# A gated linear-attention, MLP and gated-convolution kernel: a new step order, the first mask level as a product, and another place for the second phase's first split

## The reference

```python
f = 1 / (1 + exp(-f_logit))
for t in range(S):                                   # attention, per head
    state = f[:, :, t, :, None] * state + outer(k[:, :, t], v[:, :, t])
    y[:, :, t] = q[:, :, t] @ state
xn = (x - mean(x)) / sqrt(var(x) + 1e-6) * g_ln      # MLP on the 384 channels of y
x  = x + relu(xn @ w_ch1) @ w_ch2                    # 384 -> 1536 -> 384
h  = relu(x @ w_in)                                  # 384 -> 1024
gate = sigmoid(conv_w[0]*h[t-1] + conv_w[1]*h[t] + conv_w[2]*h[t+1])
out = (h * gate) @ w_out                             # 1024 -> 384
```

## Time and profile before

| | us |
|---|---|
| median of 3 runs | 750.89 |
| lowest, highest | 747.57, 751.74 |
| the profiled execution's own time | 746.53 |
| its span, first to last instruction | 744.8 |

### The profile page before, as it was taken

The page is one execution under the profiler, slowest core; times in us unless marked ns, Lnnn a source line. Parts: engine busy times, 40 slices in busy tenths (PEclk is TensorE's granted clock), DMA queues, the critical chain, the costliest instruction groups (busy, mean ns, idle before and its releaser), DMA issues.

```text
span 744.8 us, 20447 instructions
## 1 busy us (share of the span) xinstructions
PE 706.2 (95%) x8912; PEld 652.2 (88%) x8912; DVE 544.8 (73%) x1003; ACT 312.2 (42%) x604; POOL 182.2 (24%) x179
## 2 busy tenths in 40 slices
PE   3789999999999998999999999999999999999998
PEld 3556798998998998999899899999989999999997
DVE  4878989889769868858867974532577777767774
ACT  3244531431431251251143143222467776776764
POOL 8102303264154344327306414400000000000000
PEclk9758999999999999999999999999999999999999
DMA  6825601561433244073152112114310220220101
GB/s 191 196 72 151 140 3 55 157 144 55 81 148 95 41 143 140 2 181 87 56 150 85 56 55 86 54 36 151 106 54 1 74 73 1 74 70 4 37 37 37
DMA packets 22793, 62.90 MB, mean 84 GB/s; under 512 B 4240, under 2 KB 15248, under 8 KB 22704
## 3 DMA queue, kind: packets, MB, share of 16 engines
q1 hardware_dynamic: 22704, 61.60, 29.0%
HBM read 52.14 MB, written 9.45 MB: 83 GB/s over the span
## 4 chain that ended last, share of the span: by engine, by line
PE 65%; DMA 12%; DVE 10%; POOL 7%; issue 3%; SPq 2%; ACT 1%; DVEq 0%; POOLq 0%; ACTq 0%
DMA NEAR<-near 10%; PE bank L1287 9%; PE bank L1289 9%; PE bank L1288 9%; PE bank L1092 9%; PE bank L1094 8%; PE bank L1093 7%; PE bank L1004 6%; DVE AT L820 3%; DVE Q L797 2%; POOL NEAR L588 2%; POOL NEAR L603 2%; PE bank L1044 2%; POOL NEAR L590 1%; POOL NEAR L586 1%
## 5 line engine op out<-in xcount | busy, mean ns | idle before, releaser
L688 ACT ACTIVATE HHI<-bank 128x384 fp32r<-128x384 f32 x96 | 46.9, 490 | 171.3 <-PE bank L1094 171.1
L1264 DVE SCALAR_TENSOR_TENSOR TB<-HB,CW,TB 128x440 f32<-128x440 f32 x112 | 75.9, 677 | 47.0 <-ACT TB L1227 45.0
L1092 PE MATMUL bank<-HHI,W2H 128*128 128x384 f32 x288 | 103.8, 361 | 0.0
L1092 PE MATMUL bank<-XH,W1H 128*128 128x384 f32 x288 | 102.1, 355 | 0.7 <-ACT W2L L708 0.7
L1094 PE MATMUL bank<-HHI,W2L 128*128 128x384 f32 x288 | 97.4, 338 | 0.0
L1093 PE MATMUL bank<-HLO,W2H 128*128 128x384 f32 x288 | 97.0, 337 | 0.0
L1094 PE MATMUL bank<-XH,W1L 128*128 128x384 f32 x288 | 96.7, 336 | 0.0
L1093 PE MATMUL bank<-XL,W1H 128*128 128x384 f32 x288 | 96.5, 335 | 0.0
L1004 PEld LDWEIGHTS bank<-Q,K 48*64 48x64 f32 x3840 | 66.6, 145 | 30.9 <-issue 30.8
L915 DVE SCALAR_TENSOR_TENSOR HLO<-bank,HHI 128x384 fp32r<-128x384 f32 x96 | 53.2, 555 | 50.4 <-ACT HHI L688 49.3
L1004 PE MATMUL bank<-Q,K 48*64 48x32 f32 x3840 | 71.3, 229 | 18.3 <-DVE Q L797 12.6
(11 more groups left out here) (130 smaller groups left out, 1430.8 us busy)
## 6 DMA issues: line engine op xcount, KB each, us to landing
NEAR<-near SPq DMA_DIRECT2D x21, 960.0 KB, 5.0
V<-v SPq DMA_DIRECT2D x8, 576.0 KB, 9.0
x2d<-X SPq DMA_DIRECT2D x8, 576.0 KB, 4.5
F<-f SPq DMA_DIRECT2D x14, 288.0 KB, 5.1
K<-k SPq DMA_DIRECT2D x14, 288.0 KB, 5.7
Q<-q SPq DMA_DIRECT2D x14, 288.0 KB, 7.4
XB<-x2d SPq DMA_DIRECT2D x6, 663.0 KB, 5.8
out<-OB SPq DMA_DIRECT2D x6, 660.0 KB, 4.5
```

The costliest lines, as they stand in the source:

```text
L688: nc.scalar.activation(HHI[:, g % RA], ub[g % 2][:, 0:T], ACT.Relu).then_inc(hh_ready, 1)
L1092: mm(dst, ah, bh, start=start, stop=False, **kw)
L1264: nc.vector.scalar_tensor_tensor(out=TB[:, g % RB], in0=HB[:, g % RB, tap:tap + TB_], scalar=CW[:, g, tap:tap + 1], in1=TB[:, g % RB], op0 ...
```

## The change

Four things. The PERIOD list is reordered on all engines but SyncE, with the same 141 steps; START has a few steps in other places (on TensorE the first y now stands ahead of the first ktr). The first level's mask of every unit but unit 0, and the diagonal step of unit 0, are written as a product of the scores with the mask (`tensor_tensor`, multiply) and no longer as a predicated copy; the tiny memset ahead of each of these goes. In LAST the seven `wb` steps stand among the steps 14 to 42 and no longer 24 to 50, and `xb` stands eight steps earlier. TensorE's wait at the start of the second phase asks for the three pieces of W3 only; for all seven pieces it waits ahead of the first `down`.

```diff
         PERIOD = steps("""
-            hlo0 near0 up0 hhi0 up1 ktr0 hlo1 xacc0 xacc1 up2 xacc2 up3 nsum0 down0 gates0 hhi1 gates1
...
+            hhi0 up0 hlo0 near0 nsum0 up1 hlo1 xacc0 ktr0 up2 baseK0 xacc1 xacc2 hlo2 y0 down0 xadd0 up3
...
-        LAST = (up_down[:24] + merge(up_down[24:], [("wb", j) for j in range(len(nxt.WJ))])
-                + [("xb", 0), ("down", G1 - 1)] + [("xout", d) for d in range(KT)])
+        LAST = (up_down[:14] + merge(up_down[14:42], [("wb", j) for j in range(len(nxt.WJ))]) + [("xb", 0)] + up_down[42:]
+                + [("down", G1 - 1)] + [("xout", d) for d in range(KT)])
...
# self_(p): the diagonal of unit 0
-                spare = 2 * MASKED + NC + p.ahead
-                nc.vector.memset(SPARE[:, spare:spare + 1], 0.0)
...
-                        ins = nc.vector.copy_predicated(to, part.broadcast_to([HALF, p.n * NP, 2, QUARTER]), of)
+                        ins = tt(to, of, part.broadcast_to([HALF, p.n * NP, 2, QUARTER]), ALU.mult)
...
# mask(p, i)
-                    spare = st + (MASKED + NC) * p.ahead
-                    nc.vector.memset(SPARE[:, spare:spare + 1], 0.0)
+                    if st or u.first:
+                        spare = st + (MASKED + NC) * p.ahead
+                        nc.vector.memset(SPARE[:, spare:spare + 1], 0.0)
...
-                    ins = nc.vector.copy_predicated(to, part.broadcast_to([HALF, p.n * NP, QUARTER // m, m]), of)
+                    spread_mask = part.broadcast_to([HALF, p.n * NP, QUARTER // m, m])
+                    if st or u.first:
+                        ins = nc.vector.copy_predicated(to, spread_mask.bitcast(I32), of)
+                    else:
+                        ins = tt(to, of, spread_mask, ALU.mult)
...
# tensor(pe) of phase_b
-            pe.wait_ge(wbl_ready, len(carried.WJ))
+            pe.wait_ge(wbl_ready, KT)
...
                 if t.first and g == 0:
+                    pe.wait_ge(wbl_ready, len(carried.WJ))
                     pe.wait_ge(x2_ready, KT * (NU + 1))
```

More of the change, by code:

```diff
@@ L214, in phase_a @@
         VE = sb("VE", [P, NC])
-        SPARE = sb("SPARE", [P, 2 * MASKED + NC + 2])
+        SPARE = sb("SPARE", [P, 2 * MASKED + NC])
         RSTD = sb("RSTD", [P, NC])
@@ L322, in phase_a @@
         PERIOD = steps("""
-            hlo0 near0 up0 hhi0 up1 ktr0 hlo1 xacc0 xacc1 up2 xacc2 up3 nsum0 down0 gates0 hhi1 gates1
[L324 to L330, removed]
+            hhi0 up0 hlo0 near0 nsum0 up1 hlo1 xacc0 ktr0 up2 baseK0 xacc1 xacc2 hlo2 y0 down0 xadd0 up3
+            baseQ0 down1 hhi1 up4 ktok0 neary0 pT0 down2 hhi2 kv0 score0 pQ0 gates0 hlo3 up5 down3 sscale0
+            hlo4 st0 gates1 ktr1 up6 hhi3 mask0 hhi4 mask1 near1 hhi5 hlo5 nsum1 ktok1 pK1 pT1 norm0 hhi6 y1
+            neary1 hlo6 pQ1 xadd1 down4 sscale1 hhi7 norm1 xn0 up7 st1 pow0 pK2 xh0 sscale2 pT2 near2 kv1
+            score1 pow1 hlo7 neary2 xl0 up8 hhi8 mask2 xnt0 mask3 ktok2 down5 up9 down6 pQ2 nsum2 hlo8 mask4
+            ktr2 score2 hhi9 mask5 pK3 xadd2 pT3 xn1 y2 down7 pQ3 norm2 hlo9 st2 pK4 pT4 hhi10 pQ4 hlo10
+            up10 kv2 xl1 pK5 xn2 score3 pT5 up11 copy3 xh1 pQ5 hlo11 copy4 hhi11 down8 xh2 copy5 xnt1 xl2
+            pow2 pK6 score4 down9 xout0 pT6 xout1 down10 xnt2 pQ6 xout2 score5 down11
             """)
@@ L364, in phase_a @@
             score4.0 copy4.a wsub7.0 score5.a wlo6.0 score5.0 copy4.0 wsub8.0 mask3.0 copy5.a copy5.0 pQ2.0
-            baseK0.1 pQ3.a pK3.0 ktr0.0 mask5.a y0.0 mask4.0 pT3.0 ktok0.0 mask5.0 pQ3.0 pK4.a wlo7.0
+            baseK0.1 pQ3.a y0.0 mask4.0 pK3.0 ktr0.0 mask5.a pT3.0 ktok0.0 mask5.0 pQ3.0 pK4.a wlo7.0
             wsub9.0 ktr1.0 kv0.0 xadd0.0 ktok1.0 wlo8.0 wlo9.0 baseQ0.1 score0.1 pT4.a pK4.0 wsub10.0 pQ4.a
@@ L373, in phase_a @@
             down1.0 xl1.0 sscale2.0 score5.1 up4.0 pK3.1 xh2.0 down2.0 xl2.0 mask4.1 wlo15.0 pT3.1 ktr0.1
-            mask5.1 down3.0 st2.0 y0.1 pQ3.1 wlv8.0 hlo0.0 hlo1.0 hhi0.0 score0.2 pK4.1 hhi1.0 pT4.1 kv0.1
+            mask5.1 down3.0 st2.0 y0.1 pQ3.1 wlv8.0 hlo0.0 hhi0.0 hlo1.0 score0.2 pK4.1 hhi1.0 pT4.1 kv0.1
             wlv9.0 whi9.0 pQ4.1 hlo2.0 baseK0.2 down4.0 ktr1.1 wlv10.0 whi10.0 up5.0 pK5.1 pT5.1 azero0.2
             y1.1 copy3.1 whi11.0 pQ5.1 neary1.1 up6.0 baseQ0.2 hhi2.0 pK6.1 pT6.1 copy4.1 score1.2 copy5.1
-            down5.0 pQ6.1 hhi3.0 hlo3.0 wlv11.0 kv1.1 pT0.2 pQ0.2 hlo4.0 sscale0.1 hhi4.0 ktok0.1 xadd0.1
+            down5.0 pQ6.1 hhi3.0 hlo3.0 wlv11.0 hlo4.0 kv1.1 pT0.2 pQ0.2 sscale0.1 hhi4.0 ktok0.1 xadd0.1
             pK1.2 ktok1.1 hhi5.0 hhi6.0 up7.0 st0.1 hhi7.0 pT1.2 nsum1.1 pQ1.2 up8.0 down6.0 mask0.2
@@ L755, in self_ @@
                 dve.wait_ge(odd_done[p.ahead], 1)
-                spare = 2 * MASKED + NC + p.ahead
-                nc.vector.memset(SPARE[:, spare:spare + 1], 0.0)
                 for g in range(2):
                     rows = slice(HALF * g, HALF * g + HALF)
-                    part = SELF[rows, QUARTER * g:QUARTER * g + QUARTER].bitcast(I32)
+                    part = SELF[rows, QUARTER * g:QUARTER * g + QUARTER]
                     part = part.rearrange("p n two -> p two n").unsqueeze(1)
@@ L808, in mask @@
                     dve.wait_ge(score_done[p.ahead], u.count(LEVELS, st + 1))
-                    spare = st + (MASKED + NC) * p.ahead
-                    nc.vector.memset(SPARE[:, spare:spare + 1], 0.0)
+                    if st or u.first:
+                        spare = st + (MASKED + NC) * p.ahead
+                        nc.vector.memset(SPARE[:, spare:spare + 1], 0.0)
                 m = 2 << st
                 rows = slice(HALF * g, HALF * g + HALF)
-                part = MASK[rows, st, QUARTER * g:QUARTER * g + QUARTER].bitcast(I32)
+                part = MASK[rows, st, QUARTER * g:QUARTER * g + QUARTER]
                 part = part.rearrange("p (n m) -> p n m", m=m).unsqueeze(1)
```

2 lines of the change are left out of this document (1 added, 1 removed).

## The result

| | before | after |
|---|---|---|
| median, us | 750.2 (747.57 to 751.74, 4 runs) | 731.45 (729.56 to 733.2, 4 runs) |
| ratio, 95% interval | | 0.9753 [0.9715, 0.9791] |
| profiled execution, its span | 746.53, 744.8 | 733.2, 731.5 |

The change makes the kernel 2.5% faster. Timed again, with six runs of it and eleven of before, the medians were 730.56 and 749.43: 0.9743 [0.9719, 0.9768]. The forecast was 736.

What follows compares the result with a forecast made beforehand. TensorE, busy 95% of the span, was taken as the bound. The terms -4.2 - 7.1 + 2.0 + 0.8 - 5.0 - 1.2 sum to -14.7 us: 746.53 to 731.8, or 736.2 on the median's scale; range 727 to 747.

Steps and rivals of the forecast that it cites:

- Visits, -4.2: TensorE in PERIOD: fewer switches between MLP and small attention matmuls or transposes save 0.84 us a walk, 4.2 in five.
- Waits removed, -7.1: TensorE in the five walks: waits of 5.5 us for pQ 1 and 1.6 for xadd both go.
- Waits added, +2.0: TensorE at score 3 waits for VectorE's chain behind score 2, 0.4 us a walk, 2.0 in five.
- KTOK, +0.8: Walk without levels: y2 directly behind ktr2 must wait for the copy KTOK, 0.8 us once.
- Border, -1.2: Start of the second phase: the first up's 1.16 us wait for XBL goes, 1.2 us less.
- START, -5.0: START, bound first by VectorE: products for diagonal and first-level masks give 6.9 us, of which 5.0 was taken.
- The scale: Profiled execution of before lies 4.4 us below its median, so the forecast of 731.8 was put at 736.2.
- Product as dear as the copy: First-level masks and diagonal: the product costs as much as the copy, START gains about 0; 741 us, chance 0.10.
- Larger waits in the new order: PERIOD: waits of 2 us a walk in place of 0.4, slack being under 1 us; 744 us, chance 0.15.
- GpSimd's chain: PERIOD: late neary 2 stops xadd 2, kv 2 and score 3; slower than before, 754 with 4 us a walk, chance 0.08.
- Clock falls in every walk: PERIOD: longer stretches of small matmuls lower TensorE's clock each walk, 1.5 us a fall; 743 us, chance 0.09.
- START at full clock: START: TensorE, kept fed by VectorE, stays at the upper clock level and saves 9 us more; 727 us, chance 0.08.

Runs made afterwards that it cites:

- g: Changed kernel with SyncE's load of K waiting for the last ktr and that of Q for the last y, not the last kv and near step; 727.96 us, 0.9705.
- l: Kernel of g with the PERIOD list of before, all else kept; 732.75 us, ratio 0.9774.
- b: Kernel before with the diagonal and the first-level masks as products, nothing else; 736.69 us, ratio 0.9852.
- c: Kernel before with only the new LAST list and the later wait for the weight splits at the phase border; 746.63 us, ratio 0.9988.
- d: Changed kernel with the PERIOD list of before; 736.88 us, ratio 0.9848.
- j: Kernel before with SyncE's load of K waiting for the last ktr and that of Q for the last y; 741.52 us, ratio 0.9895.
- f: Changed kernel with scores 0, 1 and 3 each one MLP item later on TensorE, no longer beside kv; 773.96 us, ratio 1.0316.
- a: Kernel before with the new PERIOD list alone, masks still predicated copies; 743.26 us, ratio 0.9937.
- k: Changed kernel with 20 already fulfilled waits put on TensorE ahead of one score 0 in the first walk; 733.87 us, ratio 0.9793.

## Why the prediction was right, and where it wasn't

The direction and the main terms held, and the time was 4.6 us lower than forecast. That the forecast came so near is in part luck: one wait that was counted never came, the gaps and their clock were not counted, and these errors have opposite signs. By its own steps:

**Visits, -4.2.** Measured with the lists alone different (g against l): -3.8. Between small steps there is no extra, as taken; the reading of the Trainium skill (TensorEngine Tiling (Array Packing), Key Properties) by which only 2.1 would be saved, a drain at every change of mode, does not agree with this: kv to score takes 0.50 us with 16 matmuls in it, and kv to an MLP matmul 0.49.

**Waits removed, -7.1.** All gone. But the list and the product could each take most of it, which the text didn't say.

**Waits added, +2.0.** None. The step that failed is VectorE's chain behind score 2, "5.6 to 6.4 us". It took 5.22 (299.38, where y2 starts on TensorE, to 304.60), and TensorE's 7.1 came out as forecast (297.84 to 304.95). The sum added durations, but on VectorE a step starts before the one ahead of it has ended: from start to start xadd takes 0.48 and xn 0.39 for the 0.55 of each, and pT 3 0.16 for "a quarter to a whole pK (0.2 to 0.96)"; the handover ahead of the masks is 0.14 for 0.3. So the chain ends 0.35 us early.

**Missing from the sum: the loads.** "SyncE's list does not change, and no queue is passed by a DMA" was true and beside the point: the kv that releases the burst moved against score 5, and the last packet ahead of matmul 5281, which ends 3.1 to 4.0 us ahead of it in the profiles with the old list and the old loads (before, b, c, d), ends too late. For matmul 3375 before had nothing to spare. The gaps cost 3.4 us, and the clock in walks 3 and 4 1.9 (busy 58.42 and 58.51 where g has 57.19 and 57.86). In the trace of before walk 4 alone lost 1.8 to the clock. Together for the walks: -3.8 - 7.1 + 3.4 + 1.9 - 1.8 = -7.4 of the 8.25; l's undisturbed walks are also 0.2 to 0.4 shorter than before's, which gives the rest.

**KTOK, +0.8.** A wait of 0.68, the walk +0.61. **Border, -1.2.** -1.32. **START, -5.0.** -4.2 and -5.5 in the two profiles; four pieces of the diagonal take 2.60 us where they took 4.90. START's moved steps show no gain of their own (b ends at 142.65).

**The scale.** Against the profile of before the sum said -14.7; the two profiles of after give -13.3 and -16.4. The forecast of 736.2 came from adding to both kernels the 4.4 us by which before's profile lay under its median. That step failed, and it is most of the 4.6. Over 54 more executions of before the time follows the clock: the mean granted clock is 0.965 to 0.977 (0.975 in the profile), and the time grows by 0.95 us for each us of the time multiplied by the share of clock not granted (correlation 0.84). So its median has falls that its profile lacks. The changed kernel, at 0.979 to 0.983, lay within 1.3 us in six runs, and its second profile at 730.17 was at the median. That the waits ahead of the scores were the places where it fell is likely, and was not tested by itself; j, with shorter waits there, has a mean clock of 0.975 to 0.977 in all six executions.

**The rivals.** Product as dear as the copy: out, 0.553 us. Larger waits in the new order: out for this list, but f shows how near it is: three scores of a walk one MLP item later each cost 43 us. GpSimd's chain: not slower; its wait for the load of NEAR, which the prediction took as slack, was a cost of before. Clock falls in every walk: one fall, over the end of walk 3, in one of two profiles. START at full clock: in part. The lower clock began at 26 us and ended near 60, now it is still at the upper level to 30 and back at it near 55; windows of the second profile of after:

```profile
26.00:30.00 4.00, 1.49 (x35) 0.85 (x30) 3.94 (x10) 2.47 (x4) 0.00 (x0) 1.00 1.09 281
...
54.00:56.00 2.00, 2.00 (x43) 1.36 (x37) 1.98 (x6) 1.95 (x8) 0.00 (x0) 0.85 0.57 205
```

The Trainium skill (TensorE: Matmul & The Clock Gate, What's actually happening), by which the throttled state is the default and activity releases it, agrees with the falls behind idle stretches; but in the first row TensorE is busy for 1.49 of 4 us and keeps the upper level.

## What to carry to other kernels

Read the chain that ended last for loads, even where the list of waits names only compute: a load that stands in a queue behind others is seen by the engine that wants it and by nobody else. When a list is reordered, look at what the moved step releases in the DMA queues and on the engines that wait to overwrite what it reads, not only at what it waits for. Let each load wait for its own buffer's last reader, and not all of them for the last of all.

## What the runs showed of the hardware that was not expected

- TensorE stopped for up to 4.28 us in the middle of a step that waits for nothing, at a fixed position in its instructions, when the DMA engines were saturated (share 0.9 to 1.1), and went on 1.27 to 1.67 us after a packet of the instruction queue had ended. With the loads spread or left out it never did under the new list, and for 0.7 us at most under the old. The clock fell behind gaps of 1.82, 2.10, 3.86 and 4.28 us and not behind 1.53, 1.60 and, in a and f, 1.91 and 1.95; so the length of the gap alone doesn't tell.
- Of the masks of 64x384, a pair of predicated copies in runs of two columns took 1.92 us and a pair in longer runs 1.06, and four products with the same mask as the first took 2.06. For the diagonal's 64x512 one predicated copy took 1.316 us and one product 0.686.
- The 20 waits of k, which were fulfilled long before, took 0.63 us on TensorE, some 30 ns each.
